# Experts computed in pairs of row tiles, two experts ahead of the router's last group, logits on four column quarters, and attention's value products two steps at a time

## The chip, the cores and the metric

The kernel runs on one core of a Trainium2 chip. The metric is the device time of one execution in microseconds (us). The kernel before took 819.7 us (median of 3 runs, 819.58 to 820.21).

## The reference

Three stages in a row, all in fp32, with one output of 1536 x 512:

```python
# 1 attention: 2 x 8 heads, S = 768, D = 64; 8 global keys and a band of 96
scores = scale * q @ k.T + bias(head, distance)     # masked outside the band
a = softmax(scores);  x = a @ v                     # -> x [1536, 512]
# 2 dense gated block, d_ff 1536
xn = x / rms(x) * rms_g
x = (silu(xn @ w_gate) * (xn @ w_val)) @ w_out
# 3 eight experts, two per row, d_ff 1024
noisy = x @ w_gate2 + log1p(exp(x @ w_noise)) * noise
for each row, its two largest e:  out[row] += softmax_weight * relu(x[row] @ w1[e]) @ w2[e]
```

## The kernel before

**Precision.** A product of two fp32 matrices is made of three fp32r products: high x high, and high x low twice. Whoever writes an operand of such a product therefore writes a high half (ScalarE, a copy to fp32r) and then a low half (VectorE, the difference). Transposes, logits, scores and the value products are plain fp32.

**Attention** (L1466 to L1498 on TensorE) has 48 steps `w`. In a step TensorE turns the four probability blocks of `w` (L1439), computes the scores of step `w+3` (bias L1423, then keys of 64 rows L1427, both 256 columns wide), and then the value products of step `w-1` (`values`, L1444 to L1462), which write 64 of the array's columns for each of two heads. VectorE reduces and inverts, ScalarE takes the exponential, GpSimd scales the probabilities (L1344), and VectorE or ScalarE copy the turned blocks.

**Dense block** (`pe_moe`, L487). The 1536 rows go in three groups `g` of 512. In each, 12 chunks `c` of the hidden width have 24 up matmuls (L474) and 12 down matmuls (L504), each 512 columns wide. The rows of group `g` are turned (L513) between the ups of chunks 0 and 1 of the next group, and the logits of the group (L522: 16 products of 128 x 128 by 16 columns, in fp32) stand between the gate half and the value half of chunk 1. The router of a group (softplus L612, two largest, ranks, slots) runs on ScalarE and VectorE beside the next group, and GpSimd sends its entries to a list in DRAM (`send_entries`, L361). For the last group there is no next group: its router runs beside the first expert tiles.

**Experts** (`pe_experts`, L931). The rows of an expert are taken in tiles of 128, and a tile is one loop body for all experts: 24 up matmuls of 512 columns with the rows as the stationary operand (L938, L953), four transposes of each half of the hidden rows (L949, L967), 24 down matmuls (L973), and, before the eleventh of these, the transposes of the next tile's rows (L928). With the inputs drawn, the eight experts have 4, 3, 4, 4, 3, 3, 4 and 3 tiles, 28 in all, before as after. Two tiles of expert 0 use a short list that holds rows of the first two groups alone, so that they can start before the last group's router is done.

**Weights.** Each expert has 8 pieces of 512 KB: pieces 0 to 3 are `w1`, 4 to 7 `w2`. SyncE loads a piece into one of two buffers (`stage`) as soon as the piece two before it has been split (`sp.wait_ge(sems["wL"], i - 7)`, L327). ScalarE writes the high half (L675) and VectorE the low half (L681). The pieces of expert e+1 are split in the first two tiles of expert e, four in each, and TensorE waits for all of them once per expert (L980).

**GpSimd's queue** does for each tile, in this order (L898): copy a list entry (L874, L875), gather the rows of tile J (L879), then scatter the output of tile J-2 (L887) with an add in DRAM, wait for that to land, and shift the indices (L894, L895). So a gather is issued two tiles before its rows are used. L866 (`settle`) is a small operation ahead of each indirect DMA.

Of the kernel before, what the change touches and what calls it, by code (L numbers as in the profile page):

```python
# [11 lines left out]
P = 128  # L12
# [3 lines left out]
def attention_moe_kernel(nc, q, k, v, n_global, n_local, w_gate, w_val, w_out, rms_g,  # L16
# [48 lines left out]
    with ctx:  # L65
# [36 lines left out]
        w_rt = sb("w_rt", [P, HP, 2 * E])  # L102
# [3 lines left out]
        eidx = sb("eidx", [P, GT, E])  # L106
        tok = sb("tok", [P, NT], U32)
        base = sb("base", [P, GT + 1, E])
        scr = sb("scr", [P, 3])
# [39 lines left out]
        def expert_part(e, j, h):  # L149

            return slot_of(2 * NP2 * (e % 2) + NP2 * h + j)
# [17 lines left out]
        rows = xT[:, 0, GN:GN + DM]  # L169
        y_row = xT[:, 1, GN:GN + DM]  # L170
        hid = act_b[:].rearrange("p a n -> p (a n)")
        xe = slot_of(4 * NP2).rearrange("p (h c t) -> p h c t", h=2, c=KC)
        he = XN[:, 2 * DM:2 * DM + 2 * F2].rearrange("p (h c t) -> p h c t", h=2, c=FC2)
# [15 lines left out]
        lst = xT[:, 2, GN:GN + E * NT * 2].bitcast(U32).rearrange("p (n w) -> p n w", w=2)  # L189
        lst_a = xT[:, 2, GN + 256:GN + 256 + 2 * AHEAD].bitcast(U32).rearrange("p (n w) -> p n w", w=2)  # L190
        round_up = xT[:, 2, GN + 320:GN + 320 + E]
        short = xT[:, 2, GN + 384:GN + 385]
        idx = sb("idx", [P, 3], U32)
        gate_t = sb("gate_t", [P, 3])
# [33 lines left out]
        for name in (  # L228
# [16 lines left out]
                "const rc yt ytc lg lgr ez lnz tmp top pick posm posr rt sc cnt slots "  # L245
# [4 lines left out]
                "ahead short gath tx xeH xeL l1 rel1 th heH heL l2e ye slot scat ").split():  # L250
# [32 lines left out]
        def sp_early(sp):  # L283

            sp.dma_start(w_rt[:, :, 0:E], w_router.rearrange("(c p) e -> p c e", p=P)).then_inc(sems["const"], 16)
            sp.dma_start(w_rt[:, :, E:2 * E], w_noise.rearrange("(c p) e -> p c e", p=P)).then_inc(sems["const"], 16)
# [11 lines left out]
        def sp_moe(sp):  # L298
# [7 lines left out]
            for g in range(NG):  # L306
                if g == NG - 1:

                    sp.wait_ge(sems["rs"], NG)
                    sp.wait_ge(sems["sc"], 16 * 2 * GT * g)  # L310
                    sp.wait_ge(sems["xm"], 16 * GT * g)
                    sp.dma_start(lst_a.rearrange("p n w -> p (n w)"),
                                 slots_d.rearrange("(p n) w -> p n w", p=P)[:, 0:AHEAD]
                                 .rearrange("p n w -> p (n w)")).then_inc(sems["ahead"], 16)
# [9 lines left out]
            for e in range(1, E):  # L324
                for j in range(NP2):
# [4 lines left out]
                    if e == 1 and j == NP2 - 2:  # L330
# [3 lines left out]
                        sp.dma_start(lst.rearrange("p n w -> p (n w)"),  # L334
# [245 lines left out]
        def act_moe(act):  # L580
# [44 lines left out]
            for g in range(NG):  # L625
# [26 lines left out]
                if g == NG - 1:  # L652
                    rows_high(act, 1)
# [30 lines left out]
        def dve_moe(dve):  # L684
# [105 lines left out]
            for g in range(NG):  # L790
# [27 lines left out]
                if g == NG - 1:  # L818
                    rows_low(dve, 1)
# [899 lines left out]
```

## Time and profile before

| what | value |
|---|---|
| median of 3 runs | 819.7 us |
| the profiled execution, its own time | 820.68 us |
| its span | 819.0 us |
| busy share of the span | PE 96%, DVE 46%, ACT 41%, POOL 29% |
| chain that ended last | PE 83%, DVE 4%, SPq 3%, DMA 3%, issue 2% |
| attention, start to about 116 us | PE busy 105.88 us of 116 |
| dense block, 125 to 440 us | PE busy 314.28 us of 315 |
| last router and first tiles, 440 to 500 us | PE busy 52.29 us of 60, granted clock 0.94 |
| DMA | 75.14 MB, mean 92 GB/s |

Times in rows are microseconds from the span's start. PE is TensorE's matmul, PEld its weight load, DVE VectorE, ACT ScalarE, POOL GpSimd, SP SyncE. A matmul's recorded length includes the time through the array, so the distance between starts or between ends is what one costs in a stream. One fp32 product is recorded as two matmuls, one fp32r product or transpose as one. The prediction is made against the profiled execution, which lies 1.0 us above the median; 1.7 us of its time lie outside the span.

### The profile page before, as it was taken

To read this page: it belongs to the slowest core of one execution; us is meant where nothing else is said; L and a number is where in the kernel's file an instruction comes from. 1 tells how busy PE (TensorE), PEld (TensorE's weight loads), DVE (VectorE), ACT (ScalarE), POOL (GpSimd) and SP (SyncE) were. 2 spreads that over 40 slices of the span, in tenths; PEclk is the share of its full clock that TensorE was granted. 3 is DMA by queue.
4 is the path that set the end of the run, shared out by engine and by line. 5 is a ranking of instruction groups with operands and counts; after the bars stand their busy time and mean duration, and the time that the engine had idled before them with its cause. 6 is when DMAs were issued, how large, how long until landed. Compare 5 with 4: busy or idle time off the path is not lost.

```text
span 819.0 us, 11388 instructions
## 1 busy us (share of the span) xinstructions
PE 785.7 (96%) x4058; PEld 624.8 (76%) x4058; DVE 373.5 (46%) x674; ACT 333.2 (41%) x616; POOL 234.5 (29%) x428
## 2 busy tenths in 40 slices
PE   6999989999999999999999979999999999999993
PEld 4777657887788878888887768888888888888882
DVE  5777865542623225343254733545253354454221
ACT  4677864433251223431144532534343444443220
POOL 4478740000000300003202443334333343433331
PEclk9999999999999999999999999999999999999997
DMA  9878404410010000100135352546354364643120
GB/s 170 208 153 272 110 3 135 132 45 1 2 50 1 1 1 1 52 0 1 65 102 166 105 143 45 178 124 183 65 150 129 83 191 113 169 142 89 31 44 13
DMA packets 75874, 75.14 MB, mean 92 GB/s; under 512 B 45806, under 2 KB 53486, under 8 KB 75824
## 3 DMA queue, kind: packets, MB, share of 16 engines
q1 hardware_dynamic: 68416, 61.64, 25.5%
q0 software_dynamic: 7408, 12.88, 8.5%
q8 instruction: 26, 0.43, 0.2%
q14 instruction: 24, 0.20, 0.1%
HBM read 60.22 MB, written 14.28 MB: 91 GB/s over the span
## 4 chain that ended last, share of the span: by engine, by line
PE 83%; DVE 4%; SPq 3%; DMA 3%; issue 2%; ACT 2%; POOL 1%; POOLq 0%; ACTq 0%
PE banks L474 25%; PE banks L973 17%; PE banks L504 12%; PE banks L938 9%; PE banks L953 9%; PE banks L1427 2%; PE banks L1459 2%; PE banks L928 1%; PE banks L1439 1%; PE banks L967 1%; PE banks L949 1%; PE banks L522 1%; DMA rawv<-in_v_dram 1%; SPq L1270 1%; PE banks L1399 1%
## 5 line engine op out<-in xcount | busy, mean ns | idle before, releaser
L474 PE MATMUL banks<-XN,W_mid 128*128 128x512 f32 x552 | 135.3, 397 | 0.0
L973 PE MATMUL banks<-W_mid,XN 128*128 128x512 f32 x406 | 128.4, 405 | 0.0
L474 PEld LDWEIGHTS banks<-XN,W_mid 128*128 128x128 f32 x552 | 103.4, 188 | 25.7 <-issue 1.0
L365 POOL DMA_INDIRECT slots<-entry,slot_x x24 | 24.0, 1000 | 261.6 <-DVE slot_x L782 255.2
L1046 DVE TENSOR_TENSOR XN<-banks,XN 128x512 fp32r<-128x512 f32 x56 | 38.7, 691 | 118.7 <-ACT XN L1007 118.6
L973 PEld LDWEIGHTS banks<-W_mid,XN 128*128 128x128 f32 x406 | 74.4, 188 | 13.6
L1004 ACT ACTIVATE act_b<-banks 128x512 f32<-128x512 f32 x56 | 33.4, 597 | 109.8 <-PE banks L938 88.5
L973 PE MATMUL banks<-W,XN 128*128 128x512 f32 x240 | 77.2, 392 | 0.0
L474 PE MATMUL banks<-XN,W 128*128 128x512 f32 x288 | 73.6, 411 | 0.0
L474 PEld LDWEIGHTS banks<-XN,W 128*128 128x128 f32 x288 | 55.7, 196 | 13.5 <-issue 0.3
L599 ACT ACTIVATE HT<-act_b 128x512 fp32r<-128x512 f32 x36 | 22.8, 632 | 93.6 <-DVE act_b L703 93.6
L1344 POOL TENSOR_TENSOR prob<-prob,rinv 128x512 f32<-128x512 f32 (+1 forms) x48 | 48.8, 1016 | 41.1 <-DVE rinv L1627 41.0
L701 DVE TENSOR_TENSOR act_b<-act_b,banks 128x512 f32<-128x512 f32 x36 | 24.7, 686 | 75.7 <-ACT act_b L592 72.8
L887 POOL DMA_INDIRECT out_dram<-xT,idx x30 | 52.5, 1750 | 14.0 <-issue 14.0
L592 ACT ACTIVATE act_b<-banks 128x512 f32<-128x512 f32 x36 | 21.5, 597 | 84.2 <-PE banks L474 84.1
L973 PEld LDWEIGHTS banks<-W,XN 128*128 128x128 f32 x240 | 45.2, 188 | 9.8 <-DVE XN L1046 0.3
L1007 ACT ACTIVATE XN<-banks 128x512 fp32r<-128x512 f32 x56 | 33.5, 598 | 43.1 <-PE banks L949 21.6
L938 PE MATMUL banks<-W,W_end 128*128 128x512 f32 x180 | 46.8, 412 | 2.8 <-DVE W_end L1032 2.8
L953 PE MATMUL banks<-W,W_end 128*128 128x512 f32 x180 | 47.5, 399 | 0.0
L1519 ACT ACTIVATE prob<-banks,nmax 128x256 f32<-128x256 f32 (+1 forms) x96 | 43.1, 460 | 10.7 <-DVE nmax L1620 10.3
L938 PEld LDWEIGHTS banks<-W,W_end 128*128 128x128 f32 x180 | 35.8, 200 | 11.3 <-DVE W_end L1032 3.5
L675 ACT ACTIVATE W_mid<-stage 128x1024 fp32r<-128x1024 f32 x32 | 33.9, 1058 | 22.8 <-DMA stage<-in_moe_w_dram 21.9
(194 smaller groups left out, 1350.6 us busy)
## 6 DMA issues: line engine op xcount, KB each, us to landing
stage<-in_moe_w_dram SPq DMA_DIRECT2D x64, 512.0 KB
rawv<-in_v_dram SPq DMA_DIRECT2D x16, 192.0 KB, 3.9
out_dram<-zrow SPq DMA_DIRECT2D x1, 3072.0 KB, 12.3
moe_rows<-xT SPq DMA_DIRECT2D x12, 256.0 KB, 2.6
rawq<-in_q_dram SPq DMA_DIRECT2D x14, 192.0 KB, 3.6
rawk<-in_k_dram SPq DMA_DIRECT2D x14, 192.0 KB, 4.3
stage<-in_moe_w_gate_dram SPq DMA_DIRECT2D x4, 512.0 KB
stage<-in_moe_w_val_dram SPq DMA_DIRECT2D x4, 512.0 KB
```

Source lines behind the costliest of these rows:

```text
L474: last = nc.tensor.matmul(bank[2 * kind + n % 2][:], up_weight(kind, hw, k, c), xn[:, hx, k, :], start=(m == 0 and k == 0), stop=(m == 2 a ...
L504: last = nc.tensor.matmul(bank[4 + t][:], HT[:, n % 2, hh, t * P:(t + 1) * P], down_weight(hw, c), start=(c == 0 and m == 0), stop=(c == F ...
L675: nc.scalar.activation(expert_part(e, j, 0), stage[:, i % 2], ACT.Copy)\
L887: nc.gpsimd.indirect_dma_start(out, bass.IndirectOffsetOnAxis(ap=idx[:, 2:3], axis=0), y_row, None, bounds_check=TOK - 1, oob_is_err=False ...
L938: last = nc.tensor.matmul(bank[0][:], xe[:, hx, k, :], w1_part(e, hw, k, 0), start=(m == 0 and k == 0), stop=(m == 2 and k == KC - 1))
L953: last = nc.tensor.matmul(bank[1][:], xe[:, hx, k, :], w1_part(e, hw, k, 1), start=(m == 0 and k == 0), stop=(m == 2 and k == KC - 1))
L973: last = nc.tensor.matmul(bank[5][:], he[:, hh, k, :], w2_part(e, hw, k), start=(q == 1), stop=(q == 24))
L1004: nc.scalar.activation(hid[:, half * HALF:(half + 1) * HALF], bank[half][:], ACT.Relu)\
L1007: nc.scalar.activation(he[:, 0, 4 * half:4 * half + 4], bank[3 + half][:].rearrange("p (c t) -> p c t", c=4), ACT.Copy)\
L1046: nc.vector.tensor_tensor(he[:, 1, c], bank[3 + half][:].rearrange("p (c t) -> p c t", c=4), he[:, 0, c].bitcast(F32), ALU.subtract).then_ ...
L1344: nc.gpsimd.tensor_tensor(p, p, rinv[:, w % 4].unsqueeze(2).to_broadcast([P, 2, CW - c]), ALU.mult)\
L1519: nc.scalar.activation(prob[:, w % 3, side, c:CW], bank[w % 2 * 2 + side][:, 0:CW - c], ACT.Exp, bias=nmax[:, w % 4, side:side + 1], accum ...
```

## The change

Three parts. (1) In attention, the value products of steps w-2 and w-1 are issued together in every even step w. (2) The logits of a group are four products that stand on four 32-column quarters of the array at once, 512 columns wide, one for each quarter of the model width; ScalarE copies the result, and a second set of four small products with a selection matrix adds the quarters up. (3) Of each expert the first two tiles form a pair of 256 rows: the up product has the weights as its stationary operand and the 256 rows moving, so that its result is already turned and no hidden rows are transposed. The remaining tiles ("ones") are as before, but on their own loop; they are 1 for experts 1, 4, 5 and 7, and 2 for experts 0, 2, 3 and 6. The order is pair 0, pair 1, the one of expert 1, the two ones of expert 0, then for each expert from 2 on its pair and its ones. Both pairs 0 and 1 use short lists of the first two groups. Expert 2 uses the weight slots of expert 1, expert 3 those of expert 0. GpSimd no longer keeps shifted indices: a scatter waits for its own tile's output.

```diff
@@ expert_part: weight slots @@
-            return slot_of(2 * NP2 * (e % 2) + NP2 * h + j)
+            return slot_of(2 * NP2 * (e if e < 2 else (e + 1) % 2) + NP2 * h + j)
@@ TensorE: logits @@
-                for t in range(GT):
-                    for c in range(KC):
-                        last = nc.tensor.matmul(logit_bank(g)[:, t * 2 * E:(t + 1) * 2 * E], turned_rows(g, t)[:, c, :],
-                                                w_rt[:, c, :], start=(c == 0), stop=(c == KC - 1))
+                for c in range(KC):
+                    last = nc.tensor.matmul(bank[4][c * GW:(c + 1) * GW, :], w_cols[:, c * 2 * E:c * 2 * E + GW], xT[:, c, c0:c0 + GN],
+                                            start=True, stop=True)
+                last.then_inc(sems["lgp"], 1)
+            def logits_sum(g):
+                pe.wait_ge(sems["lgc"], g + 1)
+                for t in range(GT):
+                    last = nc.tensor.matmul(logit_bank(g)[:, t * 2 * E:(t + 1) * 2 * E], logit_parts(g)[:, t * P:(t + 1) * P], sel[:],
+                                            start=True, stop=True)
                 last.then_inc(sems["lg"], 1)
@@
                     up(pe, g + 1, 1, between=lambda: logits(g))
+                    logits_sum(g)
@@ ScalarE: softplus @@
+                act.wait_ge(sems["lgp"], g + 1)
+                nc.scalar.activation(logit_parts(g), bank[4][:], ACT.Copy).then_inc(sems["lgc"], 1)
                 act.wait_ge(sems["lg"], g + 1)
@@ GpSimd: pool_experts @@
+            def fetch_pair(i, tokens=TOK):
+                if i >= 3:
+                    pool.wait_ge(sems["turnT"], i - 2)
+                nc.gpsimd.indirect_dma_start(rows3[i % 3], None, xm[0:tokens, :],
...
+            def scatter_pair(i):
+                pool.wait_ge(sems["yT"], i + 1)
+                nc.gpsimd.indirect_dma_start(out, bass.IndirectOffsetOnAxis(ap=pair_list(i)[:, 0:1], axis=0), y3[i % 3],
...
+                pool.wait_ge(sems["scT"], 16 * (i + 1))
+            def scatter_one(ap, s, c):
+                pool.wait_ge(sems["y1"], s + 2)
+                settle(c)
+                nc.gpsimd.indirect_dma_start(out, bass.IndirectOffsetOnAxis(ap=ap, axis=0), y_one, None,
...
+                pool.wait_ge(sems["sc1"], (s + 1) * 16)
+                settle(c + 1).then_inc(sems["free1"], 1)
+            def loop_one(e, n, before):
+                with pool.Fori(first_of_loop(e), n) as t:
+                    J = before + t
+                    here, after = bass.ds(t + e * NT, 1), bass.ds(t + e * NT + 1, 1)
+                    pool.wait_ge(sems["turn1"], one_turn(e, J))
+                    nc.gpsimd.tensor_tensor(idx[:, 0:1], lst[:, here, 0], zero_i[:], ALU.add).then_inc(sems["slot"], 1)
+                    nc.gpsimd.tensor_tensor(gate_t[:], lst[:, here, 1].bitcast(F32), scr[:, 0:1], ALU.add)\
+                        .then_inc(sems["slot"], 1)
+                    nc.gpsimd.tensor_tensor(idx[:, 1:2], lst[:, after, 0], zero_i[:], ALU.add).then_inc(sems["slot"], 1)
+                    pool.wait_ge(sems["slot"], one_count(e, J) * 3)
+                    settle(1)
+                    fetch_one(idx[:, 1:2])
+                    scatter_one(idx[:, 0:1], one_index(e, J), 2)
+            for e in range(2, E):
+                n, before = tiles_of(pool, e)
+                pool.wait_ge(sems["turn1"], before + e + 1)
+                settle(7)
+                fetch_one(lst[:, e * NT + 2, 0:1])
+                if e + 1 < E:
+                    fetch_pair(2 * e + 2)
+                    fetch_pair(2 * e + 3)
+                scatter_pair(2 * e)
+                scatter_pair(2 * e + 1)
+                loop_one(e, n, before)
@@ TensorE: pe_experts @@
+            def turn_one(x, rows=rows_one):
...
+                    pe.wait_ge(sems["row1"], 16 if isinstance(x, int) and x == 0 else x * 16)
...
+            def pair(e, between, before=None):
+                pe.wait_ge(sems["xbL"], 2 * e + 2)
+                pe.wait_ge(sems["wL"], NP1 - 6 + e * NP2 + NP2 // 2)
+                for fb in range(FC2):
+                    for m, (hw, hx) in enumerate(((0, 0), (1, 0), (0, 1))):
+                        for k in range(KC):
+                            last = nc.tensor.matmul(pair_bank(fb), expert_part(e, k, hw)[:, fb * P:(fb + 1) * P],
+                                                    xe_pair[:, hx, k, :], start=(m == 0 and k == 0),
+                                                    stop=(m == 2 and k == KC - 1))
+                    last.then_inc(sems["upT"], 1)
+                    if e == 0 and fb in routing:
+                        routing[fb]()
+                pe.wait_ge(sems["wL"], NP1 - 6 + (e + 1) * NP2)
...
+                for t in range(2):
+                    q = 0
+                    for k in range(FC2):
+                        if t == 0:
+                            pe.wait_ge(sems["hbL"], FC2 * e + k + 1)
+                        for m, (hh, hw) in enumerate(PASSES):
+                            if (t, q) in between:
+                                between[t, q]()
+                            q += 1
+                            last = nc.tensor.matmul(bank[5 + t][:], he_pair[:, k, hh, t * P:(t + 1) * P],
+                                                    w2_part(e, hw, k), start=(q == 1), stop=(q == 24))
+                    last.then_inc(sems["downT"], 1)
+            def loop_one(e, n, before):
+                with pe.Fori(first_of_loop(e), n) as t:
+                    J = before + t
+                    x = one_turn(e, J)
+                    one(e, one_index(e, J), x, xe_one, {10: lambda: turn_one(x)}, max(4, 2 * e + 2))
+            pair(0, {(0, 8): row(2), (1, 8): row(3)})
+            pair(1, {(1, 8): first_ones, (1, 18): lambda: turn_one(1, rows_rest)})
+            n, before = tiles_of(pe, 1)
+            loop_one(1, n, before)
+            n, before = tiles_of(pe, 0)
+            one(0, before, 2, xe_rest, {2: row(4), 9: lambda: turn_one(before + 2), 16: row(5)}, 4)
+            loop_one(0, n, before)
+            for e in range(2, E):
+                n, before = tiles_of(pe, e)
+                between = {(1, 14): lambda: turn_one(before + e + 1)}
+                if e + 1 < E:
+                    between |= {(0, 8): row(2 * e + 2), (1, 4): row(2 * e + 3)}
+                pair(e, between, before)
+                loop_one(e, n, before)
@@ ScalarE: act_experts, experts from 2 on (VectorE follows with the low halves) @@
+            def pair_hidden(e, fb):
+                act.wait_ge(sems["upT"], FC2 * e + fb // 2 * 2 + 2)
+                nc.scalar.activation(he_pair[:, fb, 0], pair_bank(fb), ACT.Relu).then_inc(sems["hbH"], 1)
+            for e in range(2, E):
+                n, before = tiles_of(act, e)
+                for fb in range(FC2):
+                    pair_hidden(e, fb)
+                    if fb % 2 == 1:
+                        expert_high(act, e, 4 + fb // 2)
+                if e + 1 < E:
+                    pair_row_high(act, 2 * e + 2)
+                    expert_high(act, e + 1, 0)
+                    expert_high(act, e + 1, 1)
+                    pair_row_high(act, 2 * e + 3)
+                    expert_high(act, e + 1, 2)
+                one_row(before + e + 1)
+                if e + 1 < E:
+                    expert_high(act, e + 1, 3)
+                loop_one(e, n, before)
@@ VectorE: dve_experts, end of a pair @@
+                one_row(before + e + 1)
+                if e + 1 < E:
+                    expert_low(dve, e + 1, 3)
+                pair_out(2 * e + 1)
@@ TensorE: attention @@
-                    if w >= 1:
+                    if w % 2 == 0 and w >= 2:
+                        values(w - 2)
                         values(w - 1)
+                values(UB - 2)
```

## Rows read from the trace of the kernel before

**Rows 1.** Costliest groups and busy time by stage: busy us, mean ns, idle before; then windows

```profile
L1004 ACT ACTIVATE act_b<-banks 128x512 f32<-128x512 f32 x56 | 33.4, 597 | 109.8 <-PE banks L938 88.5 <-PE banks L953 20.9 <-issue 0.4
...
500.00:791.00 291.00, 290.98 (x1419) 236.81 (x1418) 123.42 (x143) 119.86 (x168) 107.98 (x238) 1.00 0.44 119
```

**Rows 2.** The chain that ended last: start us, us, what; inside three expert tiles

```profile
546.17 2.72 PE banks L938 x12
...
554.83 0.44 PE banks L928 x4
...
558.49 2.72 PE banks L938 x12
...
780.80 2.72 PE banks L938 x12
```

**Rows 3.** TensorE's waits and the clock around the first expert tiles (clock is 0.61 below)

```profile
PE banks L938 <- DVE W_end L1032: 2.8, 2, 1.4
...
482.60:487.00 4.40, 4.37 (x12) 3.46 (x13) 0.75 (x1) 0.00 (x0) 1.64 (x8) 0.61 0.13 23
```

**Rows 4.** The chain that ended last, around the logits of group 0 and group 2

```profile
233.77 3.48 PE banks L522 x32
237.24 4.44 PE banks L474 x12
...
448.61 4.43 PE banks L938 x12
```

**Rows 5.** TensorE in order of time inside one attention step, and a narrower look

```profile
62.69 0.66 PE L1439 MATMUL banks<-ident,prob 128*128 128x128 f32 x4
63.10 0.48 PE L1423 MATMUL banks<-bias,ident_r 128*128 128x256 f32 x2
63.51 0.70 PE L1427 MATMUL banks<-kT,qT 64*128 64x256 f32 x4
64.14 0.44 PE L1459 MATMUL banks<-pT,va 128*64 128x128 f32 x4
...
63.10 0.36 PE L1423 MATMUL banks<-bias,ident_r 128*128 128x256 f32 x1
```

**Rows 6.** ScalarE and VectorE in order of time: weight pieces through the two buffers

```profile
551.85 1.22 DVE L681 TENSOR_TENSOR W_mid<-stage,W_mid 128x1024 fp32r<-128x1024 f32 x1 [0.26 <-ACT W_mid L675]
...
557.39 1.06 ACT L675 ACTIVATE W_mid<-stage 128x1024 fp32r<-128x1024 f32 x1 [1.49 <-DMA stage<-in_moe_w_dram]
558.48 1.23 DVE L681 TENSOR_TENSOR W_mid<-stage,W_mid 128x1024 fp32r<-128x1024 f32 x1 [1.60 <-ACT W_mid L675]
...
563.76 1.06 ACT L675 ACTIVATE W_mid<-stage 128x1024 fp32r<-128x1024 f32 x1 [0.57 <-DMA stage<-in_moe_w_dram]
```

**Rows 7.** The nearest group to a 256-column hidden tile on ScalarE

```profile
L1533 ACT ACTIVATE xT<-banks 128x256 f32<-128x256 f32 x12 | 4.6, 387 | 6.6 <-PE banks L1459 6.6
```

**Rows 8.** A tile's output, its scatter and the next gather, in order of time

```profile
570.54 0.19 POOL L874 TENSOR_TENSOR idx<-xT,zero_i 128x1 uint32<-128x1 uint32 x1 [0.44 <-POOL gate_t L895]
...
781.03 0.75 DVE L1063 TENSOR_SCALAR xT<-banks,gate_t 128x512 f32<-128x512 f32 x1 [2.10 <-PE banks L973]
...
782.60 1.59 POOL L887 DMA_INDIRECT out_dram<-xT,idx  x1 [0.54 <-issue]
...
787.53 0.18 POOL L894 TENSOR_TENSOR idx<-idx,zero_i 128x1 uint32<-128x1 uint32 x1 [3.34 <-DMA out_dram<-xT,idx]
...
790.08 0.19 POOL L874 TENSOR_TENSOR idx<-xT,zero_i 128x1 uint32<-128x1 uint32 x1 [1.83 <-PE banks L928]
...
791.23 1.05 POOL L879 DMA_INDIRECT xT<-moe_rows,idx  x1 [0.54 <-issue]
```

**Rows 9.** The one gather that TensorE waited for, and the scatters' landing times

```profile
476.28 1.04 POOL L879 DMA_INDIRECT xT<-moe_rows,idx  x1
480.56 0.66 PE L928 MATMUL banks<-ident,xT 128*128 128x128 f32 x4 [2.72 <-DMA xT<-moe_rows,idx]
...
DMA to landing us min/median/max: 2.8/4.9/7.3
```

More of the change, by code:

```diff
@@ L844, in dve_moe, with tiles_of @@
             dve_experts(dve, ranks, counts)
-        def expert_pieces(e, t):
-            return [(e + 1, j) for j in range(4 * t, 4 * t + 4)] if e + 1 < E and t < 2 else []
-        def tiles_of(eng, e, reads=True):
+        def tiles_of(eng, e):
+            eng.wait_ge(sems["cnt"], 1)
             n = eng.value_load(cnt_i[0:1, 0, e:e + 1])
-            first = eng.value_load(cnt_i[0:1, 1, e:e + 1])
-            return n, first
+            before = eng.value_load(cnt_i[0:1, 1, e:e + 1])
+            return n, before
@@ L975, in tile @@
-                    last.then_inc(sems["l2e"], 1)
-                    if last_of_first:
-                        transpose_rows(pe, J + 2)
-            for e in range(E):
-                pe.wait_ge(sems["wL"], NP1 - 6 + (e + 1) * NP2)
-                if e == 0:
-                    for t in range(AHEAD):
-                        tile(t, e, last_positions if t == 0 else None, t == AHEAD - 1)
-                    pe.wait_ge(sems["cnt"], 1)
-                n, first = tiles_of(pe, e)
-                with pe.Fori(AHEAD if e == 0 else 0, n) as t:
-                    tile(first + t, e)
@@ L989, in rows_high @@
-        def rows_high(act, seen):
-            act.wait_ge(sems["tx"], seen)
-            nc.scalar.activation(xe[:, 0], bank[2][:].rearrange("p (c t) -> p c t", c=KC), ACT.Copy)\
-                .then_inc(sems["xeH"], 1)
-        def act_experts(act, routing):
-            def tile(J, pieces, between=None, rows_last=False):
-                if pieces:
-                    expert_high(act, *pieces[0])
-                if between is not None:
-                    between()
+                            last = nc.tensor.matmul(bank[5][:], he_one[:, hh, k, :], w2_part(e, hw, k),
+                                                    start=(q == 1), stop=(q == 24))
@@ new lines, in loop_one @@
+            def loop_one(e, n, before):
+                with act.Fori(first_of_loop(e), n) as t:
+                    J = before + t
+                    one(one_index(e, J))
+                    one_row(one_turn(e, J))
+            for fb in range(FC2):
+                pair_hidden(0, fb)
+                if fb == 3:
+                    routing()
+                if fb in (5, 7):
+                    expert_high(act, 1, (fb - 5) // 2)
+            pair_row_high(act, 2)
+            expert_high(act, 1, 2)
@@ new lines, in act_experts @@
+            expert_high(act, 1, 3)
+            pair_row_high(act, 3)
+            for fb in range(FC2):
+                pair_hidden(1, fb)
+                if fb % 2 == 1:
+                    expert_high(act, 1, 4 + fb // 2)
+            one_row(0)
+            one_row(1, xe_rest)
+            n, before = tiles_of(act, 1)
+            loop_one(1, n, before)
+            n, before = tiles_of(act, 0)
+            one(before)
+            pair_row_high(act, 4)
+            expert_high(act, 2, 0)
```

465 lines of the change are left out of this document (277 added, 188 removed).

## The prediction

> **What bounds the kernel now.** I read the costliest groups, the windows by stage, the chain, then the waits. ScalarE's hidden tiles of the experts are 56, two for each of 28 tiles, and they wait for TensorE; between 500 and 791 us TensorE is busy 290.98 of 291 us at full clock [rows 1]. In the chain a tile takes 558.49 - 546.17 = 12.32 us (12.33 below), half of its 24 ups 2.72 us (0.227 each), four transposes 0.44 (0.109 each), which leaves 0.231 for each of 24 downs; the next rows are turned 8.7 us after the tile's start [rows 2]. Nothing else is on the path, so work taken off TensorE counts in full, and a wait put in front of it counts in full. The head of the experts is the exception: waits for split rows (2.8 us) and for a gather (2.7), and twice a stretch at the half-rate clock level [rows 3, 4, 9].
>
> **Less work on TensorE.** The profiled time is 820.7, 1.0 above the median.
> - Attention. Two bias matmuls of 256 columns should take 2 x 0.12, the distance of their ends (63.58 - 63.46), yet the next group starts 0.41 us after them: changing from 128-row to 64-row tiles costs about 0.17 [rows 5]. Merged value products save one such change in each of 23 double steps, 3.9 us if TensorE sets every step. GpSimd and VectorE are close behind and double steps are uneven, so I take -2.5 (bounds -4 and +2).
> - Logits of groups 0 and 1. Now 3.48 us, and the 12 matmuls behind them take 4.44 instead of 2.80 because the clock falls to the lower level [rows 4]. Two heads' fp32 score products of 256 columns side by side take 0.63 with a mode change, 0.46 without [rows 5]; twice the columns is 0.92, and 3.7 if the four don't run together. I take 1.2 with mode changes, 0.9 for adding up (8 of the 32 small products), and 0.7 for the Exp and the copy that the next downs now wait for (two small operations of 0.2 as at 570.54 [rows 8], and hand-overs of 0.1 to 0.2). ScalarE's copy of the quarters (0.6 [rows 1]) hides behind the value half; without that cover it is 0.6 more. 3.48 + 1.64 - 2.8 = 2.3, for two groups -4.7 (bounds -7 and +3).
> - Logits of the last group: 3.48 - 1.2 - 0.9, and the slow stretch behind (4.43 for 2.72 [rows 4]): -3.1.
> - Ups of 16 tiles: 384 x 0.227 = 87.2 us become 768 of 256 columns. Bounds: half of 0.227 (87.2 in all), and 0.149, on the line between 0.109 at 128 and 0.227 at 512 columns. Taken 0.12, the shape itself [rows 5]: 92.2, +5.0.
> - Hidden transposes 16 x 8 x 0.109 = -14.0. Each loop turns a next row tile even after its last one, 36 turns for 29: 28 x 0.109 = +3.1.
> - The head: from 448.61 to 780.80 [rows 2, 4] 26 tiles take 11.6 us more than 26 x 12.33. Rank products stay (0.7), one clock loss (1.7) is counted above: -9.2. The router of the last group runs beside pair 0 instead of beside one tile; its list is first needed after pair 1's ups, and if that cover were gone the ones of experts 1 and 0 would start late by what is missing.
> Together 820.7 - 25.4 = 795.3, the time if every wait stayed hidden. The TensorE page of the Trainium skill ("Wait - 56ns, not 53.3ns?") gives columns / 2.4 GHz + 2.5 ns, an estimate of 109 ns for 256 columns where the row has 120; by it the ups would be 8 us cheaper at most.
>
> **A wait for weights that was not there.** Before, an expert's pieces are split during two tiles of the expert before. Now pieces 4 to 7 are split during the ups of the very pair that needs them, each behind hidden tiles in ScalarE's order, and TensorE waits for all of them before its first down. Count from a pair's start. The ups end at 96 x 0.12 = 11.5 us. ScalarE takes piece 5 behind hidden tiles 2 and 3, whose ups end at 5.8: 0.2 to see it (781.03 - 780.80 [rows 2, 8]), 2 x 0.39 [rows 7], start 6.8; high and low 1.06 + 1.23, done 9.1. Only this frees the buffer for piece 7. From the end of one split to the start of the next in the same buffer the rows have 557.39 - 553.07 = 4.3 and 563.76 - 559.71 = 4.05 us [rows 6]; with 4.1 piece 7 starts at 13.2 and is done at 15.6. TensorE stands for 4.1 us. The same in pairs 1 to 7 (pair 0's weights are there): 7 x 4.1 = +28.7. For the bounds, a landing 0.5 shorter or 0.9 longer: 25 and 35. It then hardly matters whether an up costs 0.114 or 0.13.
>
> **A gather behind its own tile's scatter.** Before, GpSimd gathers the rows of tile J and then waits for the output of tile J-2. Now scatter_one(s) waits for the output of tile s itself, and the gather whose rows must be turned during tile s+1 is issued only in the next loop body, behind it. From a tile's end (780.80 in the chain): output 781.03, scatter 782.60, landed and seen 787.53, 6.7 us [rows 2, 8]. Then a settle (0.25), the loop's registers (0.44 before 570.54), and from list copies to the gather 791.23 - 790.08 = 1.15 for two copies, 1.3 for three [rows 8]: it starts at 8.7. How long a gather takes to land is seen once, 480.56 - 476.28 = 4.3 from its start beside other traffic; the fastest scatter took 2.8 [rows 9]. With 3.1, between them and nearer the fast one since little else runs, it is there at 11.8; TensorE wants it at 8.7 [rows 2]. Stall 3.1 us (bounds 2.8 and 4.3), also in a loop's last body, which gathers rows that nobody uses. Behind TensorE's wait are queued the last 14 downs, the output and the next pair.
> In the first body after the pairs of experts 2 to 6 it is later. The pair ends at 15.6 + 48 x 0.231 + 12 x 0.109 = 28.0. Its second output stands on VectorE behind piece 3 of the next expert, and that behind two turns of the buffer: piece 7 done 15.6, piece 1 landed 19.7, its low half behind the first output (22.6) done 23.8, piece 3 landed 27.9, low half done 30.2, output 31.0. Its scatter is seen 3.0 + 0.6 + 4.9 = 8.5 after the pair's end (the landing is the median [rows 9]), the gather starts at 10.2 and lands at 13.3: stall 4.5.
> Over the 12 ones: five firsts and expert 0's second 26.8, experts 1 and 7 and three seconds 5 x 3.1 = 15.5, expert 0's first, with one more turn ahead of it, 2.4: +44.7.
>
> **The clock.** Some 19 stalls of 2.4 to 4.5 us are new. Before 482.6, TensorE did four transposes in about 4.9 us, and then the next matmuls ran at the half-rate level: clock 0.61 over 4.4 us [rows 3]; the shorter waits did not do this. The Trainium skill's TensorE page ("Why this matters for your kernels") also warns of idle gaps between bursts; the row agrees. I let half of the stalls cost 1.7: +16 (bounds 0 and 32).
>
> **Sum.** 795.3 + 28.7 + 44.7 + 16 = 884.7, forecast 884 us.
>
> **Rivals.**
> - Faster, nothing late: 795. It decides at one point: gather and scatter together must land within 8.7 us of a tile's end, and a buffer's turn (load, high, low) must stay below about 4.5 us. For it speaks that TensorE waited for neither after 500 us [rows 1]; against it that the scatter alone takes 6.7 and a turn 6.4. Chance 0.08.
> - Weights in time, gathers late: 795 + 12 x 3.1 + half of 12 clock losses (10) = 842. It needs loads of 512 KB to land in about 2 us. Chance 0.12.
> - Gathers in time, weights late: 795 + 28.7 + 6 = 830. It needs the add in DRAM to land much faster than in any row. Chance 0.08.
> - Attention turns slower: the turned blocks of even steps can be copied only when the double block has gone; 24 x 0.4 = 10 above the forecast, 894. Against it: VectorE does a reduction first. Chance 0.05.
> - The logits don't do what they say (one after another, or the clock falls all the same): 5 to 8 us, inside the range. The Trainium skill's tiling page ("Key Properties") says that changing the tiling mode drains the engine; that speaks against the logits and for the merged values. The 0.17 us of rows 5 agrees and is in both terms.
>
> **Numbers.** The forecast with its bounds (860 to 906) has 0.67. Faster 0.09, within 0.2% (about what a measurement of this kernel can tell from no change) 0.02, slower 0.89. The range, 828 to 904, leaves out the case of 795 and the upper tail.
>
> **What would show it.** After the change: in each pair from 1 on a gap of about 4 us between last up and first down, ended by VectorE's low split; in each of the ones a gap of 3 to 5 us before the row transposes, ended by the DMA of moe_rows, so that a one takes 15 to 17 us; granted clock below 1.00 after 500 us; full clock behind the logits of groups 0 and 1; 12 ups of a pair in 1.44 us. If the gaps before the row transposes are missing, gathers are issued earlier than I read in GpSimd's order, and the time is 40 us or more below my number; if there is none before the downs, a buffer turns faster than rows 6 say.

## The result, and the profile after

The changed kernel takes 889.6 us (median of 4 runs, 885.9 to 891.5) beside 819.6 for the kernel before on the same chip (819.5 to 820.2): ratio 1.083, 95% interval [1.080, 1.086]. The forecast was 884 us with a range of 828 to 904. The profiled execution took 885.9 us, its span is 884.1, so it stands 65.2 us above the profiled execution of before.

The page of the changed kernel: instructions and busy time, granted clock in 40 slices, the chain by engine.

```profile
span 884.1 us, 11452 instructions
PE 794.6 (90%) x4294; PEld 643.1 (73%) x4294; DVE 384.5 (43%) x716; ACT 322.0 (36%) x626; POOL 203.3 (23%) x280
...
PEclk9999999999999999999999999999889999998997
...
PE 62%; issue 11%; DMA 10%; DVE 6%; POOL 4%; ACT 4%; POOLq 1%; DVEq 0%; ACTq 0%
```

TensorE's share fell from 96% to 90% and its share of the chain from 83% to 62%. Its busy time grew by 9 us, though the change takes work off it: that is the clock, as the windows show (last numbers of a row: granted clock, DMA share, GB/s).

```profile
500.00:880.00 380.00, 315.24 (x1649) 263.64 (x1647) 130.83 (x174) 110.25 (x174) 88.12 (x128) 0.93 0.35 90
624.00:631.00 7.00, 6.24 (x17) 5.00 (x18) 1.23 (x3) 1.59 (x3) 0.00 (x0) 0.51 0.35 110
```

In [rows 1] the same stage had TensorE busy without a hole at clock 1.00. Now it is idle for a sixth of it, and at clock 0.93. The waits of TensorE (total, times, longest) name what ended the holes:

```profile
PE banks L1022 <- DMA xT<-moe_rows,idx: 31.0, 11, 4.1
PE banks L1051 <- DVE W_end L733: 16.2, 4, 5.0
PE banks L1051 <- DVE W_mid L733: 10.5, 3, 3.9
PE banks L1666 <- POOL prob L1571: 5.4, 6, 1.8
PE banks L1022 <- DMA xT<-moe_rows,xT: 1.5, 1, 1.5
```

L1022 turns the rows of a one, L1051 is a pair's first down. None of the first, second, third and fifth row is in the list of before except one gather, [rows 9]. They make 11 + 1 late gathers (32.5 us) and 7 late weights (26.7 us), all in the places that the forecast named. The fourth, GpSimd's probabilities in attention, was there before with 3.1 us; experiment 1 is about it.

**A pair's gap**, from the chain that ended last (start us, us, what):

```profile
609.35 5.77 PE banks L1031 x48
...
616.79 1.24 DVE W_mid L733
618.04 4.14 DMA stage<-in_moe_w_dram
622.21 1.06 ACT W L727
623.30 1.23 DVE W_mid L733
...
624.76 3.75 PE banks L1051 x8
```

This is the pair of expert 3. The buffer that holds piece 5 comes free at 618.04, piece 7 lands 4.14 us later, is split in 2.3, and only then does TensorE begin its downs. It had stood for 3.9 us, and the 8 downs behind it take 3.75 us instead of 1.85: the half-rate level of the clock, the window 624 to 631 above at 0.51. A turn of the buffer is as in [rows 6].

The landing is only a small part of this wait. ScalarE takes piece 7 behind its last two hidden tiles, and these need the last ups. In this pair it had done them at 621.56 and then waited 0.65 us for the landing. In the pairs of experts 4 and 5 it did not wait at all, and TensorE stood all the same (chain of the pair of expert 4):

```profile
673.76 11.52 PE banks L1031 x96
...
685.30 0.66 ACT XN L1139 x2
685.96 1.06 ACT W_mid L727
...
687.05 1.24 DVE W_end L733
...
688.52 3.42 PE banks L1051 x8
```

The last split waits for the last ups, and TensorE for the split: 3.2 us with no load in the chain. Over the seven pairs ScalarE waited 4.2 us for the landing of piece 7 (1.5 and 1.7 in the pairs of experts 1 and 2), so about 22 of the 26.7 us come from the order of ScalarE's work.

**A one's gap**, engines in order of time, around the two ones behind the pair of expert 3:

```profile
641.41 0.74 DVE L1226 TENSOR_SCALAR xT<-banks,xT 128x512 f32<-128x512 f32 x1
...
643.03 1.56 POOL L930 DMA_INDIRECT out_dram<-xT  x1 [5.79 <-DVE xT L1226]
...
648.13 0.18 POOL L958 TENSOR_TENSOR idx<-xT,zero_i 128x1 uint32<-128x1 uint32 x1 [3.54 <-DMA out_dram<-xT]
...
649.58 1.08 POOL L940 DMA_INDIRECT xT<-moe_rows,idx  x1 [0.55 <-issue]
...
652.79 0.47 PE L1022 MATMUL banks<-ident,xT 128*128 128x128 f32 x1 [3.79 <-DMA xT<-moe_rows,idx]
...
659.00 2.90 PE L1059 MATMUL banks<-W,W_end 128*128 128x512 f32 x12
...
665.57 0.18 POOL L937 TENSOR_TENSOR scr<-scr 128x1 f32<-128x1 f32 x1 [3.19 <-DMA out_dram<-xT,idx]
...
667.62 1.06 POOL L940 DMA_INDIRECT xT<-moe_rows,idx  x1 [0.56 <-issue]
...
669.83 0.66 PE L1022 MATMUL banks<-ident,xT 128*128 128x128 f32 x4 [1.95 <-DMA xT<-moe_rows,idx]
```

Second one: tile starts at 659.00, scatter seen at 665.57 (6.6 after), gather issued at 667.62 (8.6 after, forecast 8.7), and TensorE, ready before that, waits 1.95 us. First one: the pair's second output on VectorE, the scatter behind it until 648.13, the gather at 649.58, a wait of 3.79.

**Logits** of group 0, chain, from the ups before them:

```profile
234.20 0.99 PE banks L561 x8
235.19 3.00 PE banks L512 x12
238.19 0.81 PE banks L569 x8
...
239.59 3.04 PE banks L542 x12
```

Four products on four quarters take 0.99 us against 3.48 in [rows 4], and the 12 ups behind them 3.00 against 4.44: the clock stays up (granted 1.00 between 225 and 245 us, 0.91 before).

### The profile page after: what moved, and what is told of

The parts are those of the page before. It is cut to its first block, busy times and chain, and to the rows that moved or that the text cites. A ratio compares the mean times of both kernels' runs of the same rounds, so it can differ in the third digit from the quotient of the medians.

```text
span 884.1 us, 11452 instructions
## 1 busy us (share of the span) xinstructions
PE 794.6 (90%) x4294; PEld 643.1 (73%) x4294; DVE 384.5 (43%) x716; ACT 322.0 (36%) x626; POOL 203.3 (23%) x280
## 4 chain that ended last, share of the span: by engine, by line
PE 62%; issue 11%; DMA 10%; DVE 6%; POOL 4%; ACT 4%; POOLq 1%; DVEq 0%; ACTq 0%
PE banks L512 23%; PE banks L542 11%; PE banks L1051 8%; PE banks L1031 7%; DMA stage<-in_moe_w_dram 4%; DMA out_dram<-xT 4%; PE banks L1093 3%; PE banks L1654 2%; PE banks L1666 2%; PE banks L1686 2%; DMA xT<-moe_rows,idx 1%; DVE W_mid L733 1%; POOL prob L1571 1%; PE banks L1626 1%; PE banks L1650 1%
## 5 line engine op out<-in xcount | busy, mean ns | idle before, releaser
L1051 PE MATMUL banks<-W_mid,XN 128*128 128x512 f32 x240 | 79.6, 434 | 16.2 <-DVE W_end L733 16.2
L1051 PEld LDWEIGHTS banks<-W_mid,XN 128*128 128x128 f32 x240 | 48.8, 209 | 27.6 <-issue 12.2
L1093 PE MATMUL banks<-W_mid,XN 128*128 128x512 f32 x180 | 63.8, 451 | 0.0
L930 POOL DMA_INDIRECT out_dram<-xT x16 | 26.4, 1653 | 127.1 <-DVE xT L1226 122.9
L1051 PE MATMUL banks<-W,XN 128*128 128x512 f32 x128 | 44.6, 426 | 10.5 <-DVE W_mid L733 10.5
L641 ACT ACTIVATE act_b<-banks 128x512 f32<-128x512 f32 x36 | 21.5, 597 | 81.7 <-PE banks L512 81.6
L1139 ACT ACTIVATE XN<-banks 128x256 fp32r<-128x256 f32 x64 | 21.1, 382 | 73.0 <-PE banks L1031 73.0
L1031 PEld LDWEIGHTS banks<-W_end,W 128*128 128x128 f32 x384 | 46.6, 192 | 1.1 <-issue 0.8
L1031 PE MATMUL banks<-W_end,W 128*128 128x256 f32 x384 | 47.3, 284 | 0.0
L1233 DVE TENSOR_TENSOR XN<-banks,XN 128x512 fp32r<-128x512 f32 x24 | 16.6, 692 | 69.7 <-ACT XN L1147 69.7
L1031 PEld LDWEIGHTS banks<-W_end,W_mid 128*128 128x128 f32 x384 | 46.6, 192 | 0.4
L1031 PE MATMUL banks<-W_end,W_mid 128*128 128x256 f32 x384 | 46.7, 283 | 0.0
```

Of the source, the lines that this page charges most:

```text
L641: nc.scalar.activation(act_b[:, n % 2], bank[n % 2][:], ACT.Sigmoid).then_inc(sems["sig"], 1)
L930: nc.gpsimd.indirect_dma_start(out, bass.IndirectOffsetOnAxis(ap=pair_list(i)[:, 0:1], axis=0), y3[i % 3], None, bounds_check=TOK - 1, oob ...
L1031: last = nc.tensor.matmul(pair_bank(fb), expert_part(e, k, hw)[:, fb * P:(fb + 1) * P], xe_pair[:, hx, k, :], start=(m == 0 and k == 0), s ...
L1051: last = nc.tensor.matmul(bank[5 + t][:], he_pair[:, k, hh, t * P:(t + 1) * P], w2_part(e, hw, k), start=(q == 1), stop=(q == 24))
L1093: last = nc.tensor.matmul(bank[5][:], he_one[:, hh, k, :], w2_part(e, hw, k), start=(q == 1), stop=(q == 24))
```

## The experiments

Twelve kernels ran. All times are beside the kernel before on the same chip, where it took 823 to 824 us; ratios carry that out. The first four shared one chip, the next four another, the last four again one.

**1. Merged value products alone**, in the kernel before:

```diff
-                    if w >= 1:
+                    if w % 2 == 0 and w >= 2:
+                        values(w - 2)
                         values(w - 1)
+                values(UB - 2)
```

> The kernel before with one part of the change alone: value products of two steps together. The term in the prediction: 2.5 us less than before, one mode change of 0.17 us saved in each of 23 double steps and some of it given back. Rival, double steps hold up the copies of turned blocks: 5 to 10 us more. Rival, other engines set attention's pace: within 1 us of before.

Measured: 822.8 us, ratio 1.0005 [0.998, 1.003]. The null rival holds: no gain that can be measured (the interval reaches from -1.3 to +2.1 us), where the sum had -2.5. First TensorE's wait for GpSimd's probabilities (the kernel before has 3.1 us of it, in 4 waits), then the end of attention in this kernel and in the kernel before:

```profile
PE banks L1439 <- POOL prob L1344: 5.1, 6, 1.8
```

```profile
102.00:116.00 14.00, 11.81 (x96) 8.30 (x94) 9.97 (x27) 8.97 (x30) 7.10 (x6) 0.88 0.01 2
```

```profile
102.00:116.00 14.00, 12.09 (x108) 8.20 (x107) 11.51 (x31) 10.56 (x33) 7.97 (x8) 1.00 0.03 8
```

TensorE waits 2 us more for GpSimd's scaled probabilities. That this is where the saved mode changes go is read from the waits and not tested. The dip of the clock (0.88 for 1.00) is not shown to come from the merging: the kernel of experiment 6, which issues the products one step at a time again, has it too (first row), and that of experiment 11, which merges them, has not (second row).

```profile
102.00:116.00 14.00, 12.55 (x98) 8.50 (x98) 10.23 (x26) 9.27 (x30) 7.09 (x6) 0.88 0.01 2
102.00:116.00 14.00, 11.73 (x103) 8.41 (x104) 11.64 (x28) 10.64 (x34) 7.79 (x7) 1.00 0.01 2
```

**2. Weights earlier.** In the changed kernel, ScalarE and VectorE split pieces 4 and 5 ahead of the pair's hidden tiles and 6 and 7 behind tiles 3 and 5 (VectorE with the low halves alike; pair 1 too):

```diff
+                expert_high(act, e, 4)
+                expert_high(act, e, 5)
                 for fb in range(FC2):
                     pair_hidden(e, fb)
-                    if fb % 2 == 1:
-                        expert_high(act, e, 4 + fb // 2)
+                    if fb in (3, 5):
+                        expert_high(act, e, 6 + fb // 4)
```

> The changed kernel with pieces 4 and 5 of an expert split ahead of the pair's hidden tiles, 6 behind hidden tiles 2 and 3 and 7 behind 4 and 5, in place of one behind each two hidden tiles. Theory, the wait is the buffer's turn begun too late: the gaps before the first down (26.7 us in 7) shrink to 1 us each or less, the clock losses behind them go, and the time is 850 to 860 us. Rival, loading itself is the limit (8 pieces of 512 KB in a pair and its ones): the wait moves to the next pair's first piece and the time stays within 10 us of the changed kernel.

Measured: 871.4 us, ratio 1.057 [1.052, 1.061], 22 us below the changed kernel by the ratios, less than expected. TensorE's waits:

```profile
PE banks L1022 <- DMA xT<-moe_rows,idx: 34.4, 11, 5.0
PE banks L1008 <- DMA xT<-moe_rows,xT: 11.0, 5, 2.9
```

The seven waits for weights fell from 26.7 to 1.6 us, and a new one took 11 us of it: the gather of the next pair's rows (L1008), which the weights had covered, is itself late. The gathers of the ones are 3.4 us worse. The edit changes ScalarE's order and with it the start of the loads, so it takes away both parts of the wait at once.

**3. Gathers earlier.** In the changed kernel GpSimd issues the gather of the next tile as soon as the row buffer has been turned, ahead of the scatter of the tile being computed; a row set more is gathered per loop.

```diff
-                    here, after = bass.ds(t + e * NT, 1), bass.ds(t + e * NT + 1, 1)
-                    pool.wait_ge(sems["turn1"], one_turn(e, J))
+                    here, after = bass.ds(t + e * NT, 1), bass.ds(t + e * NT + 2, 1)
...
+                    pool.wait_ge(sems["turn1"], one_turn(e, J) + 1)
                     settle(1)
                     fetch_one(idx[:, 1:2])
@@ between a pair's two scatters @@
                 scatter_pair(2 * e)
+                pool.wait_ge(sems["turn1"], before + e + 2)
+                settle(10)
+                fetch_one(lst[:, e * NT + 3, 0:1])
                 scatter_pair(2 * e + 1)
```

> The changed kernel with the gather for the next tile issued right after the turn of the row before it, ahead of the scatter of the tile's own output (one gather more in each loop, whose rows nobody uses). Theory: the 11 gaps before the row transposes (31.0 us) go, with the clock losses behind them, and only the one of expert 0's first single tile stays (2 us): 845 to 855 us. Rival, the gather itself is slow and not its place: gaps stay above 1.5 us each and the time stays above 875.

Measured: 835.2 us, ratio 1.015 [1.011, 1.019]: 54 us less (56 by the ratios), more than the 35 to 45 expected. Part of the surplus is not the gathers, see experiments 9 to 12. TensorE waits for weights as in the changed kernel (24.8 us); the eleven waits for gathers are gone, and the twelfth, in expert 0's first one, stays with 2.1 us.

```profile
PE banks L1062 <- DVE W_end L733: 14.5, 4, 4.5
PE banks L1062 <- DVE W_mid L733: 10.3, 3, 3.6
```

**4. Both.** Edits 2 and 3 together.

> Both repairs together. Theory, the two waits and the clock losses that they cause are all that was lost: 800 to 812 us, faster than the kernel before, with the granted clock at 1.00 almost throughout after 500 us. Rival, the clock falls for another reason (the 256-column products, or loops): it stays near 0.93 after 500 us and the time is 825 to 835.

Measured: 816.5 us, ratio 0.992 [0.990, 0.995], some 5 us above the 800 to 812 expected. Waits, and TensorE busy and clock (0.98) between 500 and 800 us:

```profile
PE banks L1019 <- DMA xT<-moe_rows,xT: 13.2, 5, 2.9
PE banks L1062 <- DVE W_end L733: 2.3, 4, 1.5
```

```profile
500.00:800.00 300.00, 282.79 (x1582) 241.29 (x1581) 126.79 (x169) 106.05 (x169) 93.99 (x132) 0.98 0.42 112
```

Both causes are real and nearly add (ratios: 0.026 for the weights, 0.068 for the gathers, 0.090 together; the last two hold the 0.005 to 0.008 of experiments 9 to 12), and a third stands behind them: the pairs' rows, five waits of 2.6 us.

**5. A pair's first rows one expert earlier**, in the kernel of experiment 4; three buffers were there already:

```diff
                 if e + 1 < E:
-                    fetch_pair(2 * e + 2)
                     fetch_pair(2 * e + 3)
                 scatter_pair(2 * e)
+                if e + 2 < E:
+                    fetch_pair(2 * e + 4)
```

(and `fetch_pair(6)` ahead of expert 0's first `scatter_one`).

> Both repairs, and the first row tile of the next pair gathered one expert earlier, into the third of its three buffers. Theory: the third wait that the repairs uncovered (13.2 us in 5, before the pair's row transposes) goes with its three clock losses, 16 to 19 us less than with both repairs: a ratio to the kernel before of 0.970 to 0.975. Rival, GpSimd's queue is full and the wait moves to the next gather: less than 5 us gained.

Measured: 799.9 us, ratio 0.972 [0.969, 0.975], as expected. One wait of 3.4 us is left, in expert 0's first one, beside 2.0 us for weights in seven pairs.

```profile
PE banks L1035 <- DMA xT<-moe_rows,xT: 3.4, 1, 3.4
```

```profile
500.00:790.00 290.00, 279.69 (x1588) 240.25 (x1586) 127.49 (x170) 107.15 (x169) 100.11 (x136) 0.99 0.46 117
```

The last instruction of TensorE is at 784.8, so it is busy 279.7 of the 284.8 us to there, and these waits are about what is left.

**6 and 7. The value products again**, in the kernel of 5: as before the change (6), and merged up to step 36 only (7).

> As rows_early, with the value products issued one step at a time as before. If merging them costs nothing and gains nothing: within 1 us of rows_early. If the clock loss near 104 us is its doing: it is gone, and the time is 1 to 2 us lower. If merging gains 2.5 us as predicted: 2.5 us higher.

Measured: 798.1 us, ratio 0.970 [0.968, 0.973]. The clock's dip near 104 us stayed.

> As rows_early, with value products merged up to step 36 and one step at a time behind it, where no more queries and keys are turned. Theory: merging gains in the first part, where TensorE sets the pace, and loses in the last, where GpSimd's scaling does: 1.5 to 3 us less than rows_early. Rival, TensorE's mode changes are hidden everywhere: same as with the values undone.

Measured: 796.9 us, ratio 0.969 [0.966, 0.971], the lowest of all twelve. The three intervals (5, 6, 7) overlap, so which order is best stays open; what they show is that the merging is worth at most a few us either way.

**8. Logits as before the change**, in the kernel of 5 (16 products of 128 x 128 by 16 columns for each group, no sum, no copy).

> As rows_early, with the logits as 16 products of 16 columns for each group as before. By the prediction's terms 2.3 us more for each of groups 0 and 1 and 3.1 for group 2: 7 to 8 us above rows_early, with the granted clock falling again behind the logits. Rival, the clock falls for another reason: 3 us above.

Measured: 808.3 us, ratio 0.983 [0.980, 0.985], 8.4 us above rows_early. The chain at group 0:

```profile
233.79 3.54 PE banks L560 x32
237.33 4.38 PE banks L512 x12
```

The slow stretch behind the small products is back, so it belongs to them and not to the place. It does not come each time: behind those of group 1 the same kernel has

```profile
340.74 3.48 PE banks L560 x32
344.22 2.88 PE banks L512 x12
```

The four kernels with small products are before, values_alone, before_moved and this one. Of their twelve groups of logits two had no half-rate stretch at or behind the small products; no kernel with the quarters had one there. The 8.4 us have some 3 either way by the two intervals.

**9 to 12. The place of two tensors.** Comparing the chains of the kernels above, I found the dense block, which none of the edits 2 to 5 touches, at two speeds: 24 ups in 5.60 us in before, after and experiments 1 and 2, in 5.44 in experiments 3 to 8. Experiment 3 had lengthened a small tensor (`scr`) by four words. By the program's allocation that moved every tensor declared behind it, among them XN and HT, the moving operands of the dense block, from 96 bytes past a multiple of 128 in a partition (64 in the kernel before) to a multiple itself. The ups of the experts before the change, whose moving operand W_end starts at a multiple of 128, took 2.72 for 12 already [rows 2]. So: only the length of `scr` changed, in before (3 to 24 words) and in after (8 to 16); and `scr` allocated behind `act_b` in the kernels of 3 and 5, which puts XN and HT back to 64 past.

```diff
-        scr = sb("scr", [P, 3])
+        scr = sb("scr", [P, 24])
```

> The kernel before with nothing changed but the size of the small tensor scr (3 words to 24), so that XN and HT, the moving operands of the dense block, start at a multiple of 128 bytes in a partition instead of 64 past one. Placement theory: the trace of before has 24 dense ups in 5.60 us (0.2333 each, moving XN) but 12 expert ups in 2.72 us (0.2267 each, moving W_end, which starts at a multiple of 128); with XN and HT moved, all 1296 dense matmuls take 0.2267: 24 in 5.44 us and the time 8.6 us (1296 x 0.0067) below before, ratio 0.989 to 0.990. Rival (the 5.44 us of the later variants comes from another chip or from their other edits): 24 stay at 5.60 us and the ratio is 1.000.

Measured: 817.6 us, ratio 0.993 [0.991, 0.996]. One chunk of the dense block in the chain, in the kernel before and here:

```profile
244.45 5.60 PE banks L474 x24
250.05 2.76 PE banks L504 x12
```

```profile
247.35 5.44 PE banks L474 x24
252.79 2.72 PE banks L504 x12
```

> The changed kernel with scr at 16 words instead of 8, so that XN and HT start at a multiple of 128 bytes instead of 96 past one; nothing else. Placement theory: 24 dense ups in 5.44 instead of 5.60 us, 8.6 us less than the changed kernel, so about 881 us, ratio to before near 1.072; the waits of the experts as in the changed kernel (about 31 for gathers, 27 for weights). Rival: 24 stay at 5.60 us, ratio 1.083.

Measured: 887.0 us, ratio 1.078 [1.074, 1.082]; 24 ups in 5.44 us.

> gather_early with XN and HT put back where they lie in the kernel before (64 bytes past a multiple of 128), by allocating scr behind act_b. Placement theory: of the 54 us that gather_early gained on the changed kernel, 8.6 came from the place of XN and HT, so this takes 8.6 more than gather_early, ratio to before 1.024 to 1.026 (gather_early 1.0147), dense ups 5.60 us for 24. If the gather's place alone gave the 54, it is 1.015 as before.

Measured: 838.7 us, ratio 1.019 [1.016, 1.022] where gather_early has 1.015; ups 5.60.

> rows_early with XN and HT put back where they lie in the kernel before. Placement theory: 8.6 us more than rows_early, so 14 to 16 us below before, ratio 0.981 to 0.983 (rows_early 0.9717); this is then what the change is worth when nothing is late. If the place does nothing: 0.972.

Measured: 807.3 us, ratio 0.980 [0.978, 0.983] where rows_early has 0.972; ups 5.60.

The speed of the dense matmuls follows the place in all four, in both directions. In time the first and the last are clear of noise; the intervals of after_moved and gather_same_place overlap those of the kernels beside which they stand. The size was below my 8.6 us: by the ratios 5.7, 4, 3.8 and 6.9 us. I had taken the full 0.0067 us for the downs too, but they lose only 0.04 in 12 at 64 bytes past: 36 chunks x (0.16 + 0.04) = 7.2. In before_moved the clock at the head of the experts (0.91 between 440 and 500 us, 0.94 in before) took some of it back. Of the 54 us of experiment 3, an estimated 4 to 7 were the place and some 50 the gathers.

## Why the prediction was right, point by point

**The two waits are the result.** The verdict, both places and the mechanism of the gathers were as the forecast had them, that of the weights in part (below): taking away the late gathers and the late weights turns 1.083 into 0.992 (experiment 4), of which 0.005 to 0.008 are the place of two tensors, so that by these ratios the cures alone bring it to about the kernel before. Neither cure alone gives a kernel faster than before (1.015, 1.057). The rivals can be read as prices of these cures, taken from the ratios: gathers in time 830, measured 833 to 837; weights in time 842, measured 867, where the pairs' rows came late in their place (11 us), the base was 9 too low (below) and the clock stayed at 0.93.

**Weights: +28.7 forecast, 26.7 measured**, 3.1 to 5.0 a pair. A landing of 4.14, splits of 1.06 and 1.23, as the rows before had them. But the path was right only in part, and the near number owes something to luck. The forecast let the buffer's turn set the wait; in the trace ScalarE waits 4.2 us in all for that landing, and the rest, 3.2 us a pair, is the last split standing behind the last hidden tiles. So the rival with weights in time, which asked for loads of about 2 us, would not have come true by faster loads: its cure is the order, as in experiment 2. The 48 ups took 5.77 us, 0.120 each, the price taken from an attention row. The Trainium skill's page "TensorE: Matmul & The Clock Gate" ("Wait — 56ns, not 53.3ns?") gives by its formula an estimate of 109 ns for 256 columns; the measurement decides for 120.

**Gathers: +44.7 forecast, 32.5 measured.** The issue time was right (8.6 for 8.7) and two terms of the step were too large. A loop's last gather, whose rows nobody uses, was priced with a landing of 3.1 us from its start. A real one takes 2.9 to 3.2 (3.2 from 649.58 to 652.79), but this one 2.2 (667.62 to 669.83), so the seconds wait 1.8 to 2.0 instead of 3.1. And a pair's second output on VectorE comes 1.3 us after the pair's end (641.41 for 640.14), not 3.0. By the sum the end was at 28.0 us from the pair's start and the output at 31.0; here, with downs at half rate, they are at 30.9 and 32.2. In the five pairs from expert 2 to 6 the output comes 1.2 to 1.4 us behind the end, and the firsts wait 2.9 to 4.1 instead of 4.5. A one took 14.4 to 18.9 us from start to start, where the forecast had named 15 to 17.

**The clock: +16 forecast, about 22 measured.** The window of 380 us at 0.93 is worth 380 x 0.07 / 0.5 = 53 us at the half-rate level; the records show twelve such stretches after 480 us, nine of 3.4 us and three of 6.8, and one of them was there before. TensorE was busy for some 46 us of the 51, and half of that is lost. The guess "half of the stalls, 1.7 each" was short in number and in length: twelve of the 19 stalls had such a stretch behind them (the seven without it were waits of 1.5 to 3.1 us), and three of them, behind stalls of 3.8 to 4.1 us, were 6.8 long. It follows the stalls: 0.93 in after, 0.95 without the gathers' waits, 0.98 without both, 0.99 in rows_early.

**The sum with nothing late: -25.4 forecast, about -16 measured** (rows_same_place, 0.980). This is the step that failed most, and it stayed hidden because the gathers were too dear by 12. Its terms:
- Attention, -2.5 taken, no gain measured (experiment 1). In the chain the first four dense ups start at 121.04, 120.64 before. That difference alone says little: with the same attention code they start at 119.50 in before_moved, and with merged values between 119.01 (experiment 11) and 123.15 (rows_same_place, where the clock's dip near 104 is the longest). The bounds (-4 and +2) held the +0.4. I had named the cause, GpSimd close behind, and still taken a gain. The Trainium skill's page "TensorEngine Tiling (Array Packing)" ("Key Properties") has the change of mode drain the engine, which spoke for the gain; the runs show that 23 such changes fewer, at the 0.17 us of [rows 5], gave nothing that can be measured here.
- A pair, 23.93 us by my sum (96 ups 11.52, 12 transposes 1.32, 48 downs 11.09). In rows_same_place it takes 24.38, from 535.46 to 559.84: 0.26 of waiting for the last split before the first down and 0.2 more in the first eight downs. The pairs of experts 3 to 6 take 24.37 or 24.38 as well. Eight times 0.45 is 3.6 us that I had at nothing.

```profile
535.46 8.65 PE banks L1044 x72
...
547.24 2.08 PE banks L1064 x8
...
559.84 2.74 PE banks L1072 x12
```

- The gather in expert 0's first one stays late in these kernels, 2.2 us in rows_same_place. The forecast had it among the gathers (2.4).

**Logits: -7.8 forecast for three groups, 8.4 measured**, with some 3 either way, by undoing them (experiment 8). From the turn of group 0's rows to the downs it is 2.54 us less, 2.3 forecast. Here the drain of the same page of the Trainium skill is in the price (0.17 us of [rows 5]) and small beside the 2.5 us that the quarters save and the clock that they keep.

By steps: 820.7 - 16.3 (0.980 x 820.7; nothing late) + 26.7 + 32.5 + 22 = 885.6, measured 885.9. That it closes to 0.3 us is luck in part: the base, taken from a ratio with an interval of 2 us either way, still holds 2.2 us of late rows and 2.5 of waits for weights that the other terms hold too. The forecast of 884 was closer than its terms: 12 us too much on the gathers and 2 on the weights stood against 9 too little in the base and 6 in the clock.

## What to carry to other kernels

When work is made larger and queues are reordered, write down for each in-order queue what now stands ahead of each transfer; a kernel 8% slower came here from one gather issued behind its own tile's scatter and from the last weight piece split behind hidden tiles that themselves needed the last ups. Take such waits away one after another and read the list again each time, since one wait can cover the next, as the late weights covered the late rows of the next pair here. And compare a part that no edit touches between kernels: if its speed differs, the experiment changed more than it says.

## What the runs showed of the hardware that I had not expected

- The dense ups, matmuls of 512 fp32r columns, take 0.2267 us each if their moving operand XN starts at a multiple of 128 bytes in the partition and 0.2333 if it starts 64 or 96 bytes past one, 2.9% more (5.44 and 5.60 us for 24, in four kernels and their four counterparts). The dense downs, with HT moving, take 0.2267 and, at 64 past, 0.230. As stage and act_b moved along, that it is the moving operand is read from the matmuls: the expert ups, whose W_end stayed, kept 0.2267. The kernels' times moved by 0.5% to 0.8%, two of the four clear of noise.
- An indirect gather whose indices are all out of bounds (the last of a loop behind an expert's last tile) still takes 2.2 us from its start to TensorE's first transpose, as 667.62 to 669.83; one of 256 KB takes 2.9 to 3.2.
- Small products can cost the clock without any idle time: 32 records of 16 columns ran 3.5 us with TensorE busy throughout, and the 12 ups behind them took 4.4 us instead of 2.8, behind groups 0 and 1 in before [rows 4] and behind group 0 in experiment 8. Behind group 1 there, and behind group 0 in before_moved, they took 2.88. Four products of 512 columns in their place never had such a stretch behind them.
